# Five filter slots and five x slots in a spectral filter kernel, requests reordered, last pieces evacuated on VectorE

## The reference

```python
X = np.fft.rfft(x, axis=1)
F = (filt_r + 1j * filt_i)[None, :, :]
y = np.fft.irfft(X * F, n=x.shape[1], axis=1)
# layer 1
h = x @ w_in
g = np.where(h > 0.0, h, np.exp(np.minimum(h, 0.0)) - 1.0)
x = g @ w_out
# layer 2
h = x @ w_in
g = h * np.clip(h + 3.0, 0.0, 6.0) / 6.0
out = g @ w_out
```

## Time and profile before

| | us |
|---|---|
| median of 3 runs | 1116.21 |
| lowest, highest | 1115.38, 1118.57 |
| the profiled execution | 1117.79 |
| its span | 1116.0 |
| TensorE busy (matmuls) | 1101.5 (99%) |
| ScalarE busy | 769.0 (69%) |
| VectorE busy | 751.9 (67%) |
| GpSimd busy | 280.7 (25%) |

### The profile page before, as it was taken

One profiled execution on the slowest core, in us unless ns is written; L12 is line 12 of the kernel. 1 busy time (PEld: TensorE's weight loads), 2 busy tenths in 40 slices (PEclk: granted clock), 3 DMA queues, 4 the chain that ended last, 5 costly groups with the idle time before them and its releaser, 6 DMA issues.

```text
span 1116.0 us, 13377 instructions
## 1 busy us (share of the span) xinstructions
PE 1101.5 (99%) x4796; PEld 882.5 (79%) x4796; DVE 751.9 (67%) x933; ACT 769.0 (69%) x1156; POOL 280.7 (25%) x217
## 2 busy tenths in 40 slices
PE   8999999999999999999999999999999999999998
PEld 4565788888888888888888788888888888888886
DVE  5898566666667666666687866666666665665655
ACT  0445588888788888888899766665666566666654
POOL 3856402102102111111288821111111121120000
PEclk9999999999999999999999999999999999999999
DMA  9665300200200200200311200200101001000000
GB/s 283 195 196 177 132 1 1 75 1 1 74 1 1 75 1 1 75 1 1 112 38 57 93 1 1 75 1 15 61 1 37 37 1 38 37 1 1 38 1 37
DMA packets 29618, 54.98 MB, mean 49 GB/s; under 512 B 3440, under 2 KB 19696, under 8 KB 29552
## 3 DMA queue, kind: packets, MB, share of 16 engines
q1 hardware_dynamic: 22784, 42.98, 11.8%
q10 hardware_dynamic: 6768, 11.16, 2.9%
HBM read 35.61 MB, written 18.51 MB: 48 GB/s over the span
## 4 chain that ended last, share of the span: by engine, by line
PE 85%; ACT 4%; DVE 3%; DMA 3%; POOL 2%; issue 2%; SPq 0%; ACTq 0%; DVEq 0%; POOLq 0%
PE ps L471 43%; PE ps L462 13%; PE ps L461 13%; PE ps L460 13%; DMA w_raw<-w_dev 2%; PE ps L424 2%; DVE e L779 1%; ACT e L626 1%; PE ps L394 1%; ACT e L628 1%; ACT w_hi L598 1%; PE ps L402 1%; DMA x_ring<-x_dev 1%; POOL f_ring L824 1%; PE ps L411 1%
## 5 line engine op out<-in xcount | busy, mean ns | idle before, releaser
L793 DVE TENSOR_TENSOR g_lo<-e,g_hi 128x502 fp32r<-128x502 f32 (+1 forms) x288 | 277.2, 990 | 136.1 <-ACT g_hi L665 135.9
L460 PE MATMUL ps<-op_hi,w_hi 128*128 128x502 f32 x672 | 261.9, 390 | 1.6 <-ACT ps L658 1.6
L462 PE MATMUL ps<-op_lo,w_hi 128*128 128x502 f32 x672 | 261.9, 390 | 0.0
L461 PE MATMUL ps<-op_hi,w_lo 128*128 128x502 f32 x672 | 261.2, 389 | 0.0
L471 PE MATMUL ps<-g_lo,w_hi 128*128 128x502 f32 x766 | 236.8, 390 | 0.8 <-DVE g_lo L793 0.6
L471 PE MATMUL ps<-g_hi,w_hi 128*128 128x502 f32 x766 | 235.6, 389 | 0.0
L471 PE MATMUL ps<-g_hi,w_lo 128*128 128x502 f32 x766 | 234.9, 388 | 0.0
L862 POOL TENSOR_TENSOR op_lo<-op_raw,op_hi 128x1004 fp32r<-128x1004 f32 (+1 forms) x48 | 100.3, 2089 | 488.8 <-ACT op_hi L606 488.8
L471 PEld LDWEIGHTS ps<-g_lo,w_hi 128*128 128x128 f32 x766 | 143.3, 188 | 31.8 <-DVE g_lo L793 3.2
L471 PEld LDWEIGHTS ps<-g_hi,w_lo 128*128 128x128 f32 x766 | 144.1, 188 | 29.3
L471 PEld LDWEIGHTS ps<-g_hi,w_hi 128*128 128x128 f32 x766 | 143.8, 188 | 29.4 <-ACT g_hi L665 0.5
(11 more groups left out here) (73 smaller groups left out, 1154.3 us busy)
## 6 DMA issues: line engine op xcount, KB each, us to landing
op_raw<-y SPq DMA_DIRECT2D x36, 251.0 KB, 3.6
x_ring<-x_dev SPq DMA_DIRECT2D x32, 192.0 KB, 4.6
y<-ystage SPq DMA_DIRECT2D x12, 502.0 KB, 2.9
y<-ystage ACTq DMA_DIRECT2D x24, 235.0 KB, 2.8
out_dev<-ystage SPq DMA_DIRECT2D x11, 502.0 KB, 2.9
f_ring<-f_dev SPq DMA_DIRECT2D x13, 384.0 KB, 3.8
w_raw<-w_dev ACTq DMA_DIRECT2D x16, 256.0 KB, 4.3
w_raw<-w_dev SPq DMA_DIRECT2D x16, 256.0 KB, 3.0
```

The lines of the kernel that those rows point to most:

```text
L460: pe.matmul(out, w_hi[p][:, cols], hi, start=start, stop=False, skip_group_check=True)
L461: pe.matmul(out, w_lo[p][:, cols], hi, start=False, stop=False, skip_group_check=True)
L462: pe.matmul(out, w_hi[p][:, cols], lo, start=False, stop=True, skip_group_check=True).then_inc(done, 1)
L793: return dve.tensor_tensor(g_lo[:, tiles, :], e[:, tiles, :], f32(g_hi[:, tiles, :]), ALU.subtract)
```

## The change

- `XSLOTS` 8 to 5 and `FSLOTS` 3 to 5 (the same memory). With five ring slots filters 27 and 28 of the last position are found in the ring; only 29, 30 and 31 are loaded anew.
- SyncE's first requests: chunk x2 moves ahead of the back matrices, filter 1 comes behind them on SyncE (it was ScalarE's), and only filters up to 3 and chunks up to 4 are requested there; from then on filter i+4 is requested in the loop ahead of chunk i+4, for the kept filters without a wait of their own.
- Three warm-up products on TensorE for two.
- On ScalarE the evacuation and store of a piece stand ahead of the swap of the next group.
- Pieces 21 to 27 are evacuated by VectorE (`evac_end_piece`), four ahead of its first expert step and three within it, and stored by SyncE ahead of `load_xr(1)`. They count on a semaphore of their own.

```diff
--- before.py
+++ after.py
@@ -31,8 +31,8 @@
 PIECES = (J + IJ - 1) // IJ
 NPIECE = len(ORDER) * PIECES
 LAST_I = NPIECE - PIECES
-XSLOTS = 8
-FSLOTS = 3
+XSLOTS = 5
+FSLOTS = 5
 YSLOTS = 4
 MATS = ("A", "BX", "I2", "I2J", "I1")
 
@@ -205,7 +205,7 @@
         spec_ready, prod_ready, back_ready = sem("spec_ready"), sem("prod_ready"), sem("back_ready")
         signed = sem("signed")
         swap_ready, straight_ready, swapped_ready = sem("swap_ready"), sem("straight_ready"), sem("swapped_ready")
-        i_evac = sem("i_evac")
+        i_evac, end_piece_evac = sem("i_evac"), sem("end_piece_evac")
         y0_stored = [sem(f"y0_stored{k}") for k in range(YSLOTS)]
 
         w_loaded = [sem("w_loaded0"), sem("w_loaded1")]
@@ -345,29 +345,29 @@
             load_x(0)
             sp.dma_start(mat("BX"), mats_dev[:, P:2 * P]).then_inc(mat_loaded["BX"], 16)
             load_x(1)
+            load_x(2)
             sp.dma_start(mats[:, 2 * P:], mats_dev[:, 2 * P:]).then_inc(mat_loaded["back"], 16)
-            load_x(2)
+            load_f(1)
             load_x(3)
             load_f(2)
             load_x(4)
             load_f(3)
-            load_x(5)
-            load_f(4)
-            load_x(6)
-            load_f(5)
-            load_x(7)
-            load_f(6)
-            load_f(7)
             sp.wait_ge(zeroed, 2)
             sp.dma_start(y0[:, :, TOK:].rearrange("o p t -> p o t"), pad_zero[:]).then_inc(pad_stored, 16)
             for i in range(NG):
-                if KEEP_END <= i + FSLOTS - 1 < NG:
+                if i + FSLOTS - 1 < NG:
                     load_f(i + FSLOTS - 1)
                 if i and i + XSLOTS - 1 < NG:
                     load_x(i + XSLOTS - 1)
                 if i == FIRST_OP - 2:
                     sp.wait_ge(prod_ready, 3 * GROUPS)
                     load_xr(0)
+            for n in range(LAST_I, NPIECE):
+                pos, j0, nj = piece_cols(n)
+                at = ORDER[pos] % B * S + j0 * ICOL
+                sp.wait_ge(end_piece_evac, n - LAST_I + 1)
+                sp.dma_start(y0[ORDER[pos] // B, :, at:at + nj * ICOL],
+                             stage_slot(n)[:, 0:nj * ICOL]).then_inc(y0_stored[n % YSLOTS], 16)
             for s in range(2 * NS):
                 if s + 1 < 2 * NS:
                     load_xr(s + 1)
@@ -418,15 +418,17 @@
                 pe.wait_ge(back_ready, GROUPS * (pos + 1))
                 if LAST_I <= n < LAST_I + 2:
                     pe.wait_ge(spec_ready, NG)
-                elif n :
-                    pe.wait_ge(i_evac, n if n < LAST_I else n - 1)
+                elif n >= LAST_I:
+                    pe.wait_ge(end_piece_evac, n - LAST_I - 1)
+                elif n:
+                    pe.wait_ge(i_evac, n)
                 for j in range(nj):
                     last = pe.matmul(ps_i(n)[:, j * ICOL:j * ICOL + ICOL], back[:, pos % 2, j0 + j, :],
                                      mat("I1")[:, 0:ICOL], start=True, stop=True)
                 last.then_inc(i_done, 1)
 
             pe.wait_ge(zeroed, 1)
-            for _ in range(2):
+            for _ in range(3):
                 pe.matmul(ps[:, 0, :], back[:, 0, 0, :], back[:, 0, 0:4, :].rearrange("p j d -> p (j d)"),
                           start=True, stop=True)
             pe.wait_ge(mat_loaded["A"], 16)
@@ -534,7 +536,7 @@
                     if u == 0:
                         part_i(LAST_I + 3)
                 if v == 0:
-                    pe.wait_ge(i_evac, NPIECE)
+                    pe.wait_ge(end_piece_evac, PIECES)
                 if v >= 0:
                     if v and v % PAIRS == 0:
                         pe.wait_ge(out_evac[1], v // PAIRS)
@@ -630,16 +632,14 @@
                     act.activation(dst, src, ACT.Relu, bias=3.0).then_inc(ready, 1)
 
             act.dma_start(sign[:], sign_dev).then_inc(sign_loaded, 16)
-            for i in range(2):
-                c, g = group_of(i)
-                act.dma_start(f_kept[:, i].rearrange("p a n -> p (a n)"),
-                              f_dev[c // B, :, g]).then_inc(f_kept_loaded[i], 16)
+            act.dma_start(f_kept[:, 0].rearrange("p a n -> p (a n)"),
+                          f_dev[ORDER[0] // B, :, 0]).then_inc(f_kept_loaded[0], 16)
             for i in range(NG + 1):
-                if i + 1 < NG and combined(i + 1):
-                    swap_halves(i + 1)
                 n = piece_at(i - 1)
                 if n is not None:
                     evac_piece(n)
+                if i + 1 < NG and combined(i + 1):
+                    swap_halves(i + 1)
                 for p in range(PAIRS):
                     if i == w_step(p) - 2:
                         load_w(p)
@@ -656,8 +656,6 @@
                     if u:
                         act.wait_ge(m11_done, u)
                     act.copy(bank(BANK_B), bank(BANK_A)).then_inc(copy1_done, 1)
-                    if u == 0:
-                        evac_piece(LAST_I)
                 if v >= 0:
                     act.wait_ge(mpair_done, v + 1)
                     if v:
@@ -668,8 +666,6 @@
                     if u:
                         act.wait_ge(mpair_done, u)
                     act.copy(h2[:, 0, :], bank(BANK_X)).then_inc(s7_done, 1)
-                    if u == 0:
-                        evac_piece(LAST_I + 1)
                 if v >= 0:
                     act.wait_ge(m12_done, v + 1)
                     if v:
@@ -678,15 +674,10 @@
                 if u < NU:
                     act.wait_ge(p6_done, u + 1)
                     act.copy(bank(BANK_C), bank(BANK_A)).then_inc(copy2_done, 1)
-                    if u == 0:
-                        evac_piece(LAST_I + 2)
                     act.wait_ge(p2_done, u + 1)
                     if u:
                         act.wait_ge(lo11, u)
                     first_act(u, e[:, TILE11, :], bank(BANK_B), neg11, e11_ready)
-                if u == 0:
-                    evac_piece(LAST_I + 3)
-                    evac_piece(LAST_I + 4)
                 if u < NU and s + 1 < 2 * NS and PREP_AT <= p < PREP_AT + NOP:
                     operand_hi(s + 1, p - PREP_AT)
                 if u < NU:
@@ -694,8 +685,6 @@
                     if u:
                         act.wait_ge(d11_done, u)
                     act.copy(g_hi[:, TILE11, :], e[:, TILE11, :]).then_inc(hi11, 1)
-                    if u == 0:
-                        evac_piece(LAST_I + 5)
                 k = u - 2 - (NS - 1) * PAIRS
                 if 0 <= k < PAIRS:
                     weight_hi(PAIRS + k)
@@ -709,8 +698,6 @@
                     if u:
                         act.wait_ge(lo12, u)
                     first_act(u, e[:, TILE12, :], bank(BANK_C), neg12, e12_ready)
-                if u == 0:
-                    evac_piece(LAST_I + 6)
                 if p == 0 and u:
                     if u < NU:
                         evacuate(s - 1)
@@ -792,6 +779,14 @@
             def low(tiles):
                 return dve.tensor_tensor(g_lo[:, tiles, :], e[:, tiles, :], f32(g_hi[:, tiles, :]), ALU.subtract)
 
+            def evac_end_piece(n):
+                nj = piece_cols(n)[2]
+                dve.wait_ge(i_done, n + 1)
+                dve.wait_ge(y0_stored[n % YSLOTS], 16 * (n // YSLOTS))
+                dve.tensor_copy(stage_slot(n)[:, 0:nj * ICOL], ps_i(n)[:, 0:nj * ICOL]).then_inc(end_piece_evac, 1)
+
+            for n in range(LAST_I, LAST_I + 4):
+                evac_end_piece(n)
             for u in range(NU + 1):
                 v = u - 1
                 if v >= 0:
@@ -803,13 +798,19 @@
                     evacuate(2 * NS - 1)
                     break
                 second_act(u, bank(BANK_B), e[:, TILE11, :], e11_ready, m11_done)
+                if u == 0:
+                    evac_end_piece(LAST_I + 4)
                 dve.wait_ge(p5_done, u + 1)
                 dve.wait_ge(s7_done, u + 1)
                 dve.tensor_tensor(h2[:, 1, :], bank(BANK_C), h2[:, 0, :], ALU.add).then_inc(h22_done, 1)
+                if u == 0:
+                    evac_end_piece(LAST_I + 5)
                 dve.wait_ge(p4_done, u + 1)
                 dve.tensor_tensor(h2[:, 0, :], bank(BANK_A), h2[:, 0, :], ALU.add).then_inc(h21_done, 1)
                 dve.wait_ge(hi11, u + 1)
                 low(TILE11).then_inc(lo11, 1)
+                if u == 0:
+                    evac_end_piece(LAST_I + 6)
                 if u and u % PAIRS == 0:
                     evacuate(u // PAIRS - 1)
                 second_act(u, h2[:], e[:, TILE21:TILE22 + 1, :], epair_ready, mpair_done)
```

## The result

The changed kernel runs in 1109.39 us (median of 4 runs, 1107.86 to 1110.37), the kernel before on the same chip in 1117.25 (1115.38 to 1118.57). The ratio is 0.9926, with a 95% interval of 0.9912 to 0.9941: 7.9 us are gone. The forecast was 3.7. The time lies inside the stated range and more than twice as far down as its likeliest value, so the question is where the other 4 us come from.

The account below looks back on a forecast made before the run. TensorE, busy 99% of the span, was taken as the bound, with savings only ahead of 137 us. Terms 1.3 + 2.0 + 0.4 = 3.7 us off gave 1112.5 us against the median, range 1109.2 to 1115.4.

Parts of the forecast that it names:

- In later groups the swap is 0.3 us later: Transform groups after piece 0: VectorE, busy 3.1 of each 3.5 us, hides the later swap, so no cost.
- the tail's step: End of the transform: reused filters end the sign stalls, TensorE runs at 3.5 us per group; 2.0 us sooner.
- first term: Up to piece 3, start and weights included: 1.3 us gained, bounds -1.0 to +3.5.
- The start: First products on TensorE: third warm-up and earlier x1 bring 2.4 us at best, 0 at worst, lost again at group 7.
- The weights: Second weight pair ahead of group 7: asked for at 23.3, landing at 31.5 us, 1.0 us later than before.
- The line of 2.9 us and 1 us per 0.43 MB: Weight landing time from bytes requested ahead: 2.9 us plus 1 us per 0.43 MB; 8.5 us for the second pair.
- rival 2: Equal service of DMA queues: second weight pair lands at 29.5, total gain 5.7 us, 1110.5 us; chance 0.18.
- rival 3: Second weights at 33, TensorE waits over 3 us before back product 7, clock falls; 1114.8 us; chance 0.25.
- those sums ahead of 30: Sign of being wrong: GpSimd's second weight sums, expected at 31 to 32 us, come ahead of 30.
- Piece 0: Inverse transform's first piece: evacuation wait falls from 1.66 to near 1.0 us, clock stays up; 1.5 us saved.
- The hand-over: Last seven pieces moved off ScalarE, near 135 us: TensorE resumes at 136.2 instead of 136.57; 0.4 us, 0 to 0.6.
- Five x slots: Chunk requests four groups ahead, 10.5 us before use: cost 0, beginning when a landing exceeds 10 us.

Follow-up runs that it names:

- p_order: Kernel before with one edit: ScalarE evacuates and stores the piece ahead of the swap; 1114.77 us, ratio 0.9974.
- u_order: Changed kernel with the swap ahead of the evacuation again; 1115.2 us, ratio 0.9986 against the kernel before.
- p_warm: Kernel before with a third warm-up product alone; 1117.34 us, ratio 0.9997.
- u_warm: Changed kernel with two warm-up products; 1108.45 us, ratio 0.9926 against the kernel before.
- s_wait: Changed kernel with filters 8 to 12 too requested only when the product four groups earlier is done; 1105.9 us, ratio 0.9899 against the kernel before.
- p_end: Kernel before with the last seven pieces evacuated by VectorE and stored by SyncE, alone; 1117.27 us, ratio 0.9996.
- p_slots: Kernel before with five and five slots and the new request order alone; 1115.38 us, ratio 0.9984.
- p_order_slots: Kernel before with evacuation first plus the slots and requests, without third warm-up and moved last pieces; 1109.35 us, median of five executions, ratio 0.9928.
- u_reload: Changed kernel with ring filters 27 and 28 loaded and signed again; 1110.44 us, ratio 0.9946 against the kernel before.
- s_late: Changed kernel with the requests for ring filters 8 to 12 moved later in SyncE's loop; 1108.68 us, ratio 0.9919 against the kernel before.

## Why the prediction was right in sign and short in size

**The step that failed.** Two terms of the sum failed: one was put at nothing, the other too small. The first of them hides in the clause "In later groups the swap is 0.3 us later, and VectorE ... hides it." It costed the edit's order at nothing past piece 3, and the tail's step took "3.5 us per group" as TensorE's own time. It was the loop's. TensorE's own time was in the trace. Its instructions overlap, so take the distances from start to start, each where nothing holds it: a piece 1.08, an X product 0.68, a chunk 0.86, a back product 0.65, together 3.27. In the group from 51.80 the same steps make 3.57: the piece takes 1.16 and 0.22 us lie behind the back product. The check that was left out is this sum against the distance between two groups. In the traces this term is 3.3 us from piece 3 to piece 17: 0.3 us at eight of these groups, 0.2 to 0.3 at three more, hardly anything at the rest. The other is the sum's own first term, 1.3 us up to piece 3, which measures 4.0 (51.80 to 47.83): it had the second weights 1.0 us later than today, and they come 1.5 sooner, as told below. So of the 6.2 us missing in the traces 3.3 are the period, 2.7 the first term and 0.2 the tail. p_order (period 3.27) and u_order (period 3.57) show the cause from both sides. VectorE, at 3.1 us of work per group, did hide the later swap, as the step said, and follows the period down.

**The start, right in kind.** It was to be 2.4 us sooner at best and to lose that at group 7. It was 4.3 us sooner at back product 0 (10.1 for 14.4), since x1 did not have to be waited for at all, 4.0 at back product 4, and 0.1 at back product 8. p_warm and u_warm confirm that the third warm-up is worth nothing.

**The weights, right in kind, 2.5 us off in time.** The line of 2.9 us and 1 us per 0.43 MB gave 8.5 us for the second pair; it took 8.34. But the pair was asked for at 20.66, not 23.3, because TensorE was that much further, and landed at 29.0, not at 31.5. So the landing came out near rival 2's 29.5 without rival 2's cause, and the stall is of rival 3's kind, 1.97 us with the clock down where it had over 3: a pair that lands sooner can still be later for a TensorE that is further on. By the prediction's own count 1.6 MB stood ahead at 20.66 (7.75 requested, 6.13 moved), for which its line gives 7.9 us, so the request time was the wrong term and not the line. It also means that the prediction's own sign of being wrong came true, "those sums ahead of 30": they start at 29.07. s_wait shows the same dependence on the backlog. From 21.1 to 25.9 us its ScalarE queue moved 0.52 MB beside SyncE's 0.93; in the changed kernel the same 0.52 MB took from 21 to 29, beside 2.08. The Trainium skill, page "DMA: Bandwidth & Descriptors", section "Queues, rings and completion order", has each DMA engine take turns between its queue rows by packets. With equal turns the backlog on the one queue would hardly have mattered to the other, and here the pair took 8.3 us with the longer backlog and 4.8 with the shorter (asked for at 21.10).

**Piece 0, too low.** This is the first term of the sum. The wait of 1.66 us was expected at 1.0 and is gone altogether; the clock stayed up, as expected. At piece 3 the lead is 4.0 us where the first term had 1.3 with everything in it. ScalarE in order of time, for 41.74 and 42.58 before:

```profile
40.10 0.54 ACT L585 COPY ystage<-ps 128x470 f32<-128x470 f32 x1
...
41.11 0.45 ACT L592 COPY ps<-ps 64x384 f32<-64x384 f32 x1 [0.46 <-ACT ystage L585]
```

The evacuation of piece 0 comes 2.5 us sooner: 0.9 by the order, and 1.5 because the weights land 1.5 us sooner than today's instead of 1.0 later, so that nothing takes the 0.9 back. The 4.0 lie outside the stated bounds, -1.0 to +3.5, though the upper one was meant for just this case (weights sooner, wait and half rate gone). And 1.5 us of it belong to the one execution that was profiled: p_end has the kernel before's program up to there and waits as long at piece 1, but its clock stays at 1.00 and pieces 1 and 2 are 3.57 us apart for 5.04.

```profile
44.10 1.32 PE L432 MATMUL ps<-mats,back 128*128 128x94 f32 x10 [1.65 <-ACT ystage L591]
```

**The tail, right.** 2.0 forecast; 1.8 in p_slots, at the old period, and 2.2 in the changed kernel, of which part is the period's. The last transpose starts at 110.09, 9.5 us ahead of 119.55 where 3.3 were named; the difference comes from the period and the first term.

**The hand-over, right and small.** 0.4 forecast, 0.4 in the trace (9.5 to 9.9 in the table above), and not measurable alone in p_end. The stall was foreseen to end at TensorE's wait for `h`, which shows as 0.3 us.

**Five x slots** cost nothing, as said: in after TensorE never waits for x. The margin is thin, though. In p_order_slots, u_warm and s_wait TensorE waits 0.98, 0.45 and 0.60 us for a chunk near 18 us, too little to show in a median.

**The chances.** The sign was given 0.52. The range held by its lower end, 1109.2, which stood there for rival 2. The measured median of 1109.39 has not that rival's cause behind it; that the range held it is luck, since no term and no bound had the period in it.

**Still open.** The gain in the traces (9.9 us) and in the medians (7.9) differ by 2 us; the half rate at piece 1, in one execution of the kernel before and not in p_end's, may be most of it. The landings come from one profiled execution each. The stall ahead of back product 7 is in the traces of after, u_warm, u_reload and s_late with 1.97, 3.38, 2.81 and 3.11 us, followed by half rate in the first three and not in the last; how often that is so over many executions is not known.

## What to carry to other kernels

In a loop that looks bound by one engine, add up that engine's instructions for one round and compare the sum with the round's length: a busy share of 99% can hide a gap of 0.2 us that is a wait, and a loop through another engine that closes just ahead of it. On an in-order engine put first the work that hands a buffer back and is ready first, behind it what waits for the round's next product. And a load that another queue's weights must pass is worth holding back by a wait on the work, not by a place in the program, since here the queue whose waits were loose ran ahead: that one wait was worth 2 to 3 us.

## What the runs showed of the hardware

A stall's length alone does not say whether TensorE's granted clock falls behind it. After idle times of 1.66 us, 1.97 (after), 2.18 (p_order) and 2.81 (u_reload) it did, to 0.50 to 0.57 for 3 to 4 us. After 1.65 us (p_end, at the same piece as the 1.66), 2.06 (p_order, at 33.8), 2.37 (u_order, at piece 4) and 3.11 (s_late) it stayed at 1.00:

```profile
34.09 0.91 PE L415 MATMUL ps<-prod_r,mats 128*128 128x384 f32 x2 [3.11 <-DVE prod_i L724]
...
36.00:38.00 2.00, 2.00 (x6) 0.68 (x4) 1.90 (x4) 0.90 (x2) 2.00 (x3) 1.00 0.04 12
```

At the hand-over 1.92 us idle in p_slots left it at 1.00 from 133.5 to 137, and 1.90 us in p_order_slots, at the same place of a nearly equal program, brought it to a mean of 0.60 from 128 to 132. So a stall removed may be worth its own length or about twice that, in one execution as against another, which may be a part of why parts of the change are worth more in one company than in another; no run separates this. The Trainium skill, page "TensorE: Matmul & The Clock Gate", section "What's actually happening", says that the array goes to 2.4 GHz after sustained work; the durations of the start agree (0.88 us for two products at 8.9 in p_warm, 1.49 at 9.6 in p_end). Those runs show beside it that reaching the full rate 5 us sooner than the kernel before was worth nothing where a load landing 20 us later decided.
